# Moving the scaling and rotation of q from GpSimd to VectorE, with scaled q and k standing in PSUM

## The reference

```python
# attention: B, H, S, D = 4, 8, 768, 48
mag = np.sqrt(a_re**2 + a_im**2)
scale = np.minimum(mag, 0.999) / (mag + 1e-6)
a = (a_re + 1j*a_im) * scale                # complex decay for each position and feature
for t in range(S):
    S_re, S_im = decayed state (times a[t]) + outer(k[t], v[t]) in the real part
    y[t] = q[t] @ S_re
# mixture of experts: 3072 tokens of 384, 8 experts of width 1024, the best one of each token
out[mask] = gate_w * sigmoid(x @ w_output_gate)[e] * (relu(x[mask] @ w1[e]) @ w2[e])
# feed-forward: 384 -> 2048 -> 384 with a leaky relu of slope 0.01
```

## Time and profile before

| | |
|---|---|
| time, median of 3 runs | 1134.59 us (1134.08 to 1134.94) |
| the profiled execution | 1130.78 us, span 1129.0 us |
| TensorE busy with matmuls over the span | 973.2 us (86%) |
| VectorE, ScalarE, GpSimd busy | 482.2, 429.5, 543.7 us |
| attention (all 24 chunks) | from the start to about 361 us |
| first expert block | from 417 us on |

### The profile page before, as it was taken

How to read it: one execution, slowest core, us unless ns; L and a number is a source line. 1 busy time by engine, 2 the same in 40 slices (tenths; PEclk the granted TensorE clock), 3 DMA queues, 4 the chain that set the end, 5 groups by cost and what they waited for, 6 DMA issues and landing times.

```text
span 1129.0 us, 17090 instructions
## 1 busy us (share of the span) xinstructions
PE 973.2 (86%) x5810; PEld 850.4 (75%) x5811; DVE 482.2 (43%) x689; ACT 429.5 (38%) x697; POOL 543.7 (48%) x367
## 2 busy tenths in 40 slices
PE   2668888878987008999999999999999999999996
PEld 0556666666776007999998989899999999999996
DVE  4766888887763613443444434221211212212110
ACT  6656666666652101222222222333333333333322
POOL 3553666555541683535756399324324243242433
PEclk9868999999798558999999999999999999999999
DMA  5122234222000433234334445200001010000000
GB/s 195 59 78 69 73 107 147 71 72 71 22 1 16 172 122 134 92 103 153 124 106 132 139 146 175 50 15 29 22 15 36 15 36 15 15 29 1 28 1 29
DMA packets 45141, 82.24 MB, mean 73 GB/s; under 512 B 22917, under 2 KB 34329, under 8 KB 42521
## 3 DMA queue, kind: packets, MB, share of 16 engines
q1 hardware_dynamic: 39704, 46.81, 13.4%
q0 software_dynamic: 5376, 34.63, 8.7%
HBM read 65.80 MB, written 15.59 MB: 72 GB/s over the span
## 4 chain that ended last, share of the span: by engine, by line
PE 56%; POOL 4%; issue 3%; DVE 2%; DMA 1%; ACT 0%; SPq 0%; DVEq 0%; POOLq 0%
PE bank L1818 18%; PE bank L1831 17%; PE bank L1798 9%; PE bank L1776 8%; POOL wm L1577 2%; PE bank L1786 2%; DMA x_b<-x_sorted 1%; POOL wm L1575 1%; PE bank L1763 1%; DVE x_b L1690 1%; PE bank L1808 1%; DVE wm L1421 0%; POOL out L1601 0%; SPq L1498 0%; DVE h_tr L1704 0%
## 5 line engine op out<-in xcount | busy, mean ns | idle before, releaser
L1595 POOL TENSOR_TENSOR act_r<-act_f,act_r 128x512 fp32r<-128x512 f32 x96 | 124.7, 1298 | 259.9 <-ACT act_r L1654 256.6
L1831 PE MATMUL bank<-w_out_r,act_r 128*128 128x384 f32 x1152 | 217.7, 337 | 0.3 <-POOL act_r L1595 0.3
L1818 PE MATMUL bank<-x,w_in_r 128*128 128x512 f32 x864 | 216.7, 395 | 0.0
L1831 PEld LDWEIGHTS bank<-w_out_r,act_r 128*128 128x128 f32 x1152 | 204.8, 188 | 8.9 <-POOL act_r L1595 0.6
L1720 DVE TENSOR_TENSOR act_f<-bank,small 128x512 f32<-128x512 f32 x96 | 66.5, 692 | 292.7 <-ACT small L1651 275.2
L1818 PEld LDWEIGHTS bank<-x,w_in_r 128*128 128x128 f32 x864 | 159.6, 188 | 29.5
L1776 PE MATMUL bank<-wm,x_tr 128*128 x522 | 129.5, 402 | 3.8 <-DVE x_tr L1697 2.0
L1651 ACT ACTIVATE small<-bank 128x512 f32<-128x512 f32 x96 | 57.5, 599 | 191.3 <-PE bank L1818 191.2
L1798 PE MATMUL bank<-wm,h_tr 128*128 x696 | 128.0, 338 | 0.9 <-DVE h_tr L1704 0.9
L1798 PEld LDWEIGHTS bank<-wm,h_tr 128*128 128x128 f32 x696 | 119.5, 188 | 1.4 <-issue 1.4
L1776 PEld LDWEIGHTS bank<-wm,x_tr 128*128 128x128 f32 x522 | 97.8, 192 | 24.9 <-issue 4.9
(11 more groups left out here) (173 smaller groups left out, 1458.1 us busy)
## 6 DMA issues: line engine op xcount, KB each, us to landing
stage<-moe_w POOLq DMA_DIRECT2D x12, 1536.0 KB, 7.0
qkv_in<-in_qkv SPq DMA_DIRECT2D x24, 576.0 KB, 5.8
a_in<-in_a SPq DMA_DIRECT2D x11, 768.0 KB, 5.0
stage<-moe_w SPq DMA_DIRECT2D x4, 1536.0 KB, 7.8
x_b<-x_sorted SPq DMA_DIRECT2D x30, 193.0 KB, 2.6
y_sorted<-y_b SPq DMA_DIRECT2D x29, 192.0 KB, 1.9
xg<-y_sorted SPq DMA_DIRECT2D x24, 192.0 KB, 2.4
stage<-w_out POOLq DMA_DIRECT2D x2, 1536.0 KB, 7.1
```

The lines of the kernel that those rows point to most:

```text
L1595: pool.tensor_tensor(a[:, 1, :], act_f[f % 2][:, :], a[:, 0, :].bitcast(F32), ALU.subtract).then_inc(s_gl, 1)
L1818: last = pe.matmul(h_bank[f % 2][:, :], w_in_r[:, wp, t * F2 + f * P:t * F2 + (f + 1) * P], window_part(w, xp)[:, t, :], start=(t == 0 and ...
L1831: last = pe.matmul(o_bank[j][:, 0:W], a[:, ap, j * P:(j + 1) * P], w_out_r[:, wp, f * W:(f + 1) * W], start=(f == 0 and n == 0), stop=(f = ...
```

## The change

Scaled k and scaled q are no longer written back over `qkv_in` in SBUF but into two PSUM banks of their own (`kh_bank`, `qh_bank`), and VectorE does the scaling and the rotation of both. The banks come from the transposes: queries of both halves share one bank, and so do keys. `scale` and `rotate` of chunk `n+1` stand together in iteration `n`; scaling used to be done three chunks ahead. GpSimd keeps `cosine_log`, `sine_eps`, `carry_in`, `decay`. ScalarE takes the first half's key copy (`first_key`) and, in even iterations, `out_copy` from VectorE. Three buffers instead of two hold `fall` and `rise`. The order of the lists of ScalarE, VectorE and TensorE in the loop is changed too. Its core:

```diff
-    qt_bank, kt_bank = (bank[0], bank[2]), (bank[1], bank[3])
+    qt_bank, kt_bank, kh_bank, qh_bank = bank[0], bank[1], bank[2], bank[3]
+    FALLS = 3
@@ GpSimd, loop n = 3..24 @@
+                for m in summed(n):
+                    carry_in(m)
                 u = chain_exp(n)
                 if u is not None:
                     cosine_log(u)
                     sine_eps(u)
-                rotate_q(n + 1)          # carry_in stood before it (even n) or behind it (odd n)
                 decay(n - 1)
-                for m in summed(n):
-                    scale_q(m)
@@ VectorE @@
-                dve.tensor_tensor(k_in, k_in, rise[m % 2][:, :], ALU.mult).then_inc(s_ke, 1)
+            def scale(m):
...
+                need(dve, s_kr, 2 * m)
+                dve.tensor_tensor(kh_bank[:, 0:W], qkv_in[m % RING][:, 1, :], rise[m % FALLS][:, :],
+                                  ALU.mult).then_inc(s_ke, 1)
+                dve.wait_ge(s_fall, m + 1)
+                need(dve, s_qr, 2 * m)
+                dve.tensor_tensor(qh_bank[:, 0:W], qkv_in[m % RING][:, 0, :], fall[m % FALLS][:, :],
+                                  ALU.mult).then_inc(s_qe, 1)
+            def rotate(n):
+                # four tensor_tensor: k with sine, q with sine, k with cosine, q with cosine;
+                # in0 in kh_bank or qh_bank, in1 in SBUF; the third waits for the cosine
...
+            def second_key(n):           # key(n, 1); ScalarE has first_key(n) = key(n, 0)
@@ VectorE, loop @@
+                add_update(n - 1)
+                if n % 2 == 1:
+                    out_copy(n - 1)      # for even n it is on ScalarE, first in its iteration
                 mask(n, 0)
+                second_key(n)
+                scale(n + 1)
+                rotate(n + 1)
+                # even n: mask(n, 1), cap, phases, decay_log, half_tangent
+                # odd n:  turns, mask(n, 1), left_half, sum_squares, phases, numerator
@@ ScalarE, loop @@
+                # even n: out_copy(n-1), query(n, 1), rows(n-1), falls, epsilon, cosine_tanh, rounded,
+                #         query(n+1, 0), first_key(n+1)
+                # odd n:  falls, sine, query(n, 1), rows(n-1), phase_size, cosine, angle, squares,
+                #         load of the logs' table, query(n+1, 0), first_key(n+1), rounded, logs
@@ TensorE, transposes(n, h) @@
-                need(pe, s_qt, 2 * n + h - 1)
-                need(pe, s_kt, 2 * n + h - 1)
+                need(pe, s_qt, 2 * n + h)
+                need(pe, s_kt[1 - h], n + h)
@@ TensorE, loop, even n @@
                 scores(n, 1)
+                outputs(n, 0)
                 sum_turns(m)
-                outputs(n, 0)
                 transposes(n + 1, 0)
-                sum_logs(m + 1)
                 outputs(n, 1)
+                sum_logs(m + 1)
```

More of the change, by code:

```diff
@@ L172, in attention @@
     cosv = [sb(ctx, f"cos{i}", [P, 2 * W]) for i in range(2)]
-    fall = [sb(ctx, f"fall{i}", [P, W]) for i in range(2)]
-    rise = [sb(ctx, f"rise{i}", [P, W]) for i in range(2)]
+    fall = [sb(ctx, f"fall{i}", [P, W]) for i in range(FALLS)]
+    rise = [sb(ctx, f"rise{i}", [P, W]) for i in range(FALLS)]
     qr = [sb(ctx, f"qr{i}", [P, H, 2, D]) for i in range(2)]
@@ L232, in attention @@
     s_qt = sem("q_t_ready")
-    s_kt = sem("k_t_ready")
+    s_kt = [sem(f"k_t{i}_ready") for i in range(2)]
     s_sc = sem("scores_done")
@@ L240, in attention @@
     s_clear = sem("output_bank_cleared")
-    s_xtc = sem("x_t_ready")
+    s_xtc = [sem(f"x_t_ready{i}") for i in range(2)]
     s_lg = sem("logits_done")
@@ L315, in chunk_end @@
                 sp.wait_ge(s_fall, m + 1)
[L316 removed]
+                sp.dma_start(ends[m], fall[m % FALLS][P - 1:P, :]).then_inc(s_row, 16)
                 sp.wait_ge(s_row, 16 * m + 16)
@@ L445, in _ @@
                 cosine_log(u)
-                if n == 2:
-                    rotate_q(3)
                 sine_eps(u)
+                decay(n - 1)
+            for n in range(3, NCH + 1):
                 for m in summed(n):
[L450 to L455, removed]
+                    carry_in(m)
                 u = chain_exp(n)
@@ L611, in _ @@
             for n in range(3, NCH + 1):
[L612 to L617, removed]
-                    query(n, 1)
[L619 to L625, removed]
@@ L626, in _ @@
-                if chain_exp(n) is None:
-                    query(n, 1)
[L628 to L635, removed]
-                    query(n + 1, 0)
[L637 to L640, removed]
+                if n % 2 == 0:
+                    u = chain_exp(n)
+                    out_copy(n - 1)
+                    query(n, 1)
+                    rows(n - 1)
+                    for m in summed(n):
+                        falls(m)
+                    if u is not None:
+                        epsilon(u)
+                        cosine_tanh(u)
+                    for m in summed(n):
+                        rounded(m)
+                    query(n + 1, 0)
+                    first_key(n + 1)
+                else:
+                    for m in summed(n):
+                        falls(m)
+                    u = chain_trig(n)
+                    if u is not None:
+                        act.preload_act_table_set("trig_and_small")
+                        sine(u)
+                    query(n, 1)
+                    rows(n - 1)
+                    if u is not None:
+                        phase_size(u)
+                        cosine(u)
+                    u = chain_angle(n)
+                    if u is not None:
+                        angle(u)
+                    u = chain_log(n)
+                    if u is not None:
+                        squares(u)
+                        act.preload_act_table_set("natural_log")
+                    query(n + 1, 0)
+                    first_key(n + 1)
+                    for m in summed(n):
+                        rounded(m)
+                    if u is not None:
+                        logs(u)
@@ L777, in _ @@
             sum_squares(2)
-            for m in range(2):
-                scale_k(m)
-            rotate_k(0)
+            scale(0)
+            rotate(0)
             numerator(2)
-            key(0, 0)
             cap(2)
+            scale(1)
             mask(0, 0)
-            key(0, 1)
+            rotate(1)
+            second_key(0)
             decay_log(2)
-            rotate_k(1)
             half_tangent(2)
@@ L1006, in _ @@
                         sum_turns(m)
-                else:
-                    for m in summed(n + 1):
-                        sum_logs(m)
                 if n == NCH - 2:
@@ L1015, in _ @@
                 outputs(n, 1)
+                if n % 2 == 0:
+                    for m in summed(n + 1):
+                        sum_logs(m)
 def attention_any(sem, new, in_a, in_qkv, bank, ident, wg, flag, x_all, lg_all):
```

158 lines of the change are left out of this document (75 added, 83 removed).

## The result

The changed kernel takes 1103.3 us in the median (1102.29 to 1104.41), the kernel before 1134.34 beside it: ratio 0.9726, 95% interval 0.971 to 0.9743, 31 us less. The forecast was 1104. Its profiled execution took 1103.91 us, span 1101.9, against 1130.78 and 1129.0 of before; the spans differ by 27.1 only, mostly because the profiled execution of before was a good one: it lies 3.6 us under its median. The time of before varies: 56 further runs, on three chips, took 1130.4 to 1147.6 us.

What follows compares the result with a forecast made beforehand. No engine is full: chains through several engines set the 27.10 us pair of iterations. Eight pairs at 24.0 us save 30.4 us, filling and tail 0, so 1134.6 - 30.4 = 1104.2 us; own range 1098 to 1110, stated range 1091 to 1118.

Steps and rivals of the forecast that it cites:

- Odd part: From `falls` in the odd iteration to the next even iteration's scores, ScalarE's chain: 13.46 us to fall to 11.8.
- the logs at -2.85: Odd part, ScalarE: logs move behind query and key copies, so their wait and the two logs go, -2.85 us.
- The added rows: Odd part, ScalarE: rows now stand ahead of the phase sizes and the cosine, adding an estimated 0.52 us.
- the cosine rotations ahead of `turns`: Odd part, VectorE: `turns` behind two cosine rotations, about 1.0 us after the cosine ends, +0.25 us.
- Even part: Rest of the pair, 13.64 us before: TensorE's own list of 11.41 us plus waits, forecast 12.2 us.
- the three waits: Even part, TensorE: 0.1 us for `phases`, 0.25 for `falls`, about 0.45 for `decay_log`.
- VectorE's price: Each added scaling or rotation on VectorE taken at 0.47 us, bounded above by 1.1; 72 operations more.
- Filling: Start up to iteration 3: less contention against ScalarE's key copies and a later output copy, set at 0, bounds -1.5 and +2.
- the last of my signs of being wrong: Forecast wrong if filling to iteration 3 ends over 2 us later than 93.3.
- The falling clock: Rival: TensorE's clock keeps falling each pair, about 1.6 us lost; pair 25.6, gain 17.6 us, 1117; chance 0.24.
- the slower rival: Even iterations: ScalarE's output copy behind the logs comes 4.5 us late; pair 28.5, +5.6 us, 1140; chance 0.07.
- The better rival: Waits for `decay_log`, key copy and `phases` vanish, clock stays up; pair 22.6, -41.6 us, 1093; chance 0.15.

Runs made afterwards that it cites:

- loaded kernels: Changed kernel with GpSimd's old load put back as unused products, rotations from PSUM: 1121.21 us (0.984); the same with scaled q and k in SBUF: 1133.0 (0.9952).
- run with the angle first: Changed kernel with ScalarE's start list reordered, angle and squares of units 2 and 3 ahead of chunk 1's query and key copies: 1098.4 us (0.9662).
- kernel with logs first: Changed kernel with ScalarE's two logs ahead of the query and key copies again in odd iterations: 1125.76 us (0.9909).

## Why the prediction was right

*Bound and place.* The pair of iterations was the right unit, and TensorE's list with two chains was what set it. -30.4 us was forecast for the eight pairs, -32.6 measured. Two misses hide in that: seven pairs are 0.8 us shorter than the 24.0 forecast (5.7 us together), and the first, for which I took 24.0 as for the rest, is 3.55 us longer, at a granted clock of 0.81.

*Odd part.* 11.8 forecast, 11.74 measured. Its largest term, the logs at -2.85, was measured apart only as 1.76 in the full change. The rest fits their wait of 1.18 us for the sum of squares, which the move of q removes by itself: with only q moved, ScalarE's logs wait 0.3 us in all from 122 to 300 us, where in the kernel before they wait 8.3. The added rows, the cosine rotations ahead of `turns` and the first key copy are all where they were put: `turns` starts 0.97 us after the cosine ends (176.91 to 177.88).

*Even part.* 12.2 forecast, 11.45 measured. TensorE's own steps were right (21.2 for the pair, 21.14 measured); mis-sized were the three waits, 0.8 us together, which are not there. In particular `decay_log`, charged with up to 0.9, is over when `sum_logs` is due.

*VectorE's price.* 0.47 us a step was right: two rotations follow each other by 0.47 us and each takes 537 to 558 ns; the scaling into PSUM, the price that no row showed, is 553. The Trainium skill ("VectorE: DVE Perf Modes", section on the TRN2 errata) gives 58 fixed cycles for a source in SBUF and 120 for one in PSUM. The trace shows no such step: L723 takes 543 ns at least from PSUM, and before L724 took 543 at least from SBUF; the measurement decides. The upper bound of 1.1 us was never needed.

*The reason for it* was only half right. I wrote that the rotations are safe because they have a PSUM operand. They are, as the loaded kernels show for one of the four, but in the changed kernel they don't need it. GpSimd is busy 8.90 us a pair, not under 8 as I had written.

*Filling: the term that was off.* It was set at 0 with bounds -1.5 and +2; the trace says +4.9, and so the last of my signs of being wrong came true. Of this 2.8 us are there when the angle starts (43.64 for 40.85), and by the runs above these are the clock in the two executions and not the change. The other 2.1 us come behind it: half a microsecond by the place of the copy, and at the second place both are slow, but the changed kernel's transposes stay slow to 91.7 us and those of before only to 87.6, so part of it is the clock again. What is left for the change itself is 2 us at most (an estimate from one execution of each), at the edge of my bounds. The run with the angle first was meant to undo a delay by the change; it takes 4.9 us off the median, but what it undoes was in the kernel before too, where the angle stood behind the same query.

*The total* is in part luck. In the profiled executions the sum is -32.6 + 4.9 + 0.6 = -27.1, and against the forecast of 1100.4 the changed kernel took 1103.91, 3.5 us over. The medians agree within 1 us because I had carried the 3.8 us between median and profiled execution of before over to the changed kernel, whose median lies 0.6 us under its profiled one: these 4.4 us cover the miss.

*Rivals.* The falling clock came in the first pair only, and its price was right: 1.6 forecast a pair, 1.6 to 1.7 measured in the kernel with logs first. The slower rival, an output copy on ScalarE late behind the logs, did not: in the even iteration ScalarE's copy (184.89, 0.59 us) ends at 185.48, and the logits start at 185.68 with no wait. The margin is 0.20 us, as thin as the 0.15 that I had. The better rival was at 22.6 a pair; 23.19 lies between it and the forecast.

## What to carry to other kernels

Moving work off an engine that lengthens another's operations can pay twice, by the shorter queue and by the other engine's faster operations; here the move of q alone gave 20 of the 31 us (23 against the kernel before on its own chip), and how the two ways share it was not separated. Before a long operation beside a neighbour is blamed for a slower kernel, lay it beside the same operation in the faster one, and look at the granted clock: the same move of the logs was worth 1.76 us a pair with the other lists arranged for it and cost 1.75 without, and what it cost lay in 9 us of TensorE at half the clock, not on VectorE. And the filling of a pipeline wants its own walk: one in-order copy waiting ahead of an early chain step, in the kernel before as well as in the changed one, cost 5 us, as much as a quarter microsecond in each of twenty iterations; and two fillings are compared only after a look at where the clock was low in each.

## What the runs showed of the hardware

A clock fall can be free. In the kernel with q on VectorE and the old orders, pairs of clock 0.93 and of clock 1.00 take the same 25.55 us. TensorE catches up at its next waits: 0.57 us for the q rotation and 0.94 for `phases` in the pair at 1.00 are none and 0.48 in a pair at 0.93.

```profile
173.32:198.87 25.55, 21.38 (x194) 17.31 (x194) 21.75 (x34) 17.83 (x28) 8.90 (x6) 1.00 0.38 132
198.87:224.42 25.55, 22.60 (x194) 18.24 (x194) 21.75 (x34) 17.83 (x28) 8.91 (x6) 0.93 0.27 79
```

The granted clock in the records reads 1.00 from 10 to 50 us, although the scores at 36.41 above take 2.04 us, the time of the lower level; in the filling the durations have to be read, not that column. The contention is mutual. GpSimd's carry of 384 elements in one partition takes 0.99 us with VectorE idle (at 137.03 in the loaded kernel) and 1.70 beside VectorE's sum of squares (181.03 in the timeline above). Beside the left half one of the two is lengthened, and not always the same: in the changed kernel the carry takes 0.99 us and the left half 1.03 to 1.04 in most pairs (0.99 and 1.82 in one), and with q and logs moved they take 1.78 and 0.55 in some pairs (at 178.85 and 179.23).
